# A float32 attention and gated MoE kernel: q and k loaded with their depth in rows, and four low parts of the output weights moved in VectorE's queue

## What is computed

```python
scores = q @ k.transpose(0, 1, 3, 2) / sqrt(D)           # 32 heads, 576 x 576
x      = log1p(abs(i - j)) / log1p(max(i, 1))
bias   = maximum(x[..., None] @ w1 + b1, 0) @ w2         # one bias matrix per head, same for all batches
attn   = softmax(scores + bias)
x      = (attn @ v).transpose(0, 2, 1, 3).reshape(2304, 512)
gate   = sigmoid(x @ w_gate)
out    = (gate * (x @ w_val)) @ w_out
```

## Time and profile before

| | |
|---|---|
| time, median of 3 runs | 765.59 us (764.82 to 766.67) |
| time of the profiled execution | 765.62 us |
| its span, first to last instruction | 763.5 us |
| granted TensorE clock, mean | 0.998 |
| PE busy | 737.0 us, 97% |
| PEld busy | 604.1 us, 79% |
| DVE busy | 508.6 us, 67% |
| ACT busy | 459.0 us, 60% |
| POOL busy | 354.2 us, 46% |
| chain that ended last | PE 84%, DVE 9%, issue 3%, ACT 3%, DMA 1% |

### The profile page before, as it was taken

The page is one execution under the profiler, slowest core; times in us unless marked ns, Lnnn a source line. Parts: engine busy times, 40 slices in busy tenths (PEclk is TensorE's granted clock), DMA queues, the critical chain, the costliest instruction groups (busy, mean ns, idle before and its releaser), DMA issues.

```text
span 763.5 us, 14723 instructions
## 1 busy us (share of the span) xinstructions
PE 737.0 (97%) x5104; PEld 604.1 (79%) x5104; DVE 508.6 (67%) x1082; ACT 459.0 (60%) x939; POOL 354.2 (46%) x483
## 2 busy tenths in 40 slices
PE   7788999999999999999989999999999999999998
PEld 4336777777777767679878998999899889989996
DVE  6996777777777777756950787687068677714851
ACT  6996676776767767657632674375166437615720
POOL 0003454454457787884627562655055265603500
PEclk9999999999999999999999999999999999999999
DMA  6898133232262332113330124222011412200102
GB/s 165 195 217 174 48 80 78 66 77 71 63 200 70 81 77 50 33 44 127 111 110 1 56 83 140 82 60 80 1 57 56 165 59 81 76 8 29 55 4 80
DMA packets 92953, 63.16 MB, mean 83 GB/s; under 512 B 60496, under 2 KB 86224, under 8 KB 92880
## 3 DMA queue, kind: packets, MB, share of 16 engines
q1 hardware_dynamic: 92448, 62.13, 29.7%
q10 hardware_dynamic: 432, 0.09, 0.1%
HBM read 42.15 MB, written 9.44 MB: 68 GB/s over the span
## 4 chain that ended last, share of the span: by engine, by line
PE 84%; DVE 9%; issue 3%; ACT 3%; DMA 1%; POOL 0%; ACTq 0%; DVEq 0%; POOLq 0%
PE f_ps L1421 20%; PE z_ps L1350 18%; PE v_ps L1312 10%; PE y_ps L1350 9%; PE so_ps L1248 7%; DVE feats L942 6%; PE x_ps L1350 4%; PE ty_ps L1261 4%; PE tx_ps L1273 3%; PE so_ps L1243 2%; ACT probs L769 1%; PE tx_ps L1290 1%; PE v_ps L1192 1%; PE ty_ps L1202 1%; PE tx_ps L1278 1%
## 5 line engine op out<-in xcount | busy, mean ns | idle before, releaser
L1350 PE MATMUL z_ps<-xc,wc 128*128 128x384 f32 x864 | 165.3, 336 | 0.2
L588 POOL TENSOR_SCALAR probs<-probs,recip 128x512 f32<-128x512 f32 x128 | 89.2, 697 | 152.3 <-DVE recip L996 152.3
L1350 PEld LDWEIGHTS z_ps<-xc,wc 128*128 128x128 f32 x864 | 150.6, 188 | 3.8 <-ACT keep L796 1.9
L769 ACT ACTIVATE probs<-neg_scores,neg_max 128x576 f32<-128x576 f32 x144 | 111.1, 771 | 61.5 <-DVE neg_max L976 61.5
L976 DVE CUSTOM_DVE_ANT_0 neg_scores<-so_ps,bias 128x576 f32<-128x576 f32 x128 | 91.9, 755 | 3.7 <-PE so_ps L1231 3.2
L614 POOL TENSOR_TENSOR wc<-t_raw,wc 128x512 fp32r<-128x512 f32 x37 | 49.1, 1326 | 88.5 <-ACT wc L788 88.5
L1421 PE MATMUL f_ps<-wo_h,h_h 128*128 128x512 f32 x216 | 85.2, 394 | 2.8 <-issue 2.8
L1350 PE MATMUL y_ps<-xc,wc 128*128 128x384 f32 x432 | 86.7, 335 | 1.0 <-DVE sig L1052 0.5
L1421 PE MATMUL f_ps<-wo_l,h_h 128*128 128x512 f32 x216 | 84.9, 393 | 0.0
L1421 PE MATMUL f_ps<-wo_h,h_l 128*128 128x512 f32 x216 | 84.8, 393 | 0.0
L796 ACT ACTIVATE keep<-z_ps 128x384 f32<-128x384 f32 x108 | 52.9, 490 | 52.4 <-PE z_ps L1350 51.3
(11 more groups left out here) (124 smaller groups left out, 1491.2 us busy)
## 6 DMA issues: line engine op xcount, KB each, us to landing
w_stage<-in_w_gate SPq DMA_DIRECT2D x18, 512.0 KB, 3.6
w_stage<-in_w_val SPq DMA_DIRECT2D x18, 512.0 KB, 3.5
bias<-bias_rows SPq DMA_DIRECT2D x12, 576.0 KB, 6.5
out<-out_sb SPq DMA_DIRECT2D x18, 256.0 KB, 2.0
q_raw<-in_q SPq DMA_DIRECT2D x32, 128.0 KB, 2.8
k_raw<-in_k SPq DMA_DIRECT2D x32, 128.0 KB, 2.6
v_main<-in_v SPq DMA_DIRECT2D x32, 128.0 KB, 2.3
x_whole<-attn_transposed SPq DMA_DIRECT2D x9, 384.0 KB, 4.9
```

The source lines that it names most:

```text
L588: nc.gpsimd.tensor_scalar(row[:, 0:NT * P], row[:, 0:NT * P], by, 1.0, ALU.mult, ALU.mult).then_inc(normed, 1)
L769: nc.scalar.activation(probs[s % RING][:, place, :], neg_scores[:, place, :], ACT.Exp, bias=neg_max[:, stat(s, place)], scale=-1.0, accum_ ...
L1350: last = nc.tensor.matmul(quad_ps[bank][n % 2][:, 0:CH], wc[:, n % 2, wl, W_PARTS.index(wp), t, :], xc[:, X_PARTS.index(x), xl, t, :], sta ...
```

## The change

q and k are laid out anew in DRAM: one array `qk` with, for each of the 16 pairs, 128 rows (the depth of the first head, then of the second) of 1216 columns: 576 of k, 128 of q's last rows (64 for each head, zeros in the other head's columns), 512 of q's other rows. One DMA a pair (`load_qk`, 608 KB, rows of 4864 bytes) brings it into `qk_whole`, which lies at the place of `qk_l`. Nothing is turned on TensorE: the three `turn_` functions and all waits on them, and on the PSUM tiles that they shared, are gone. ScalarE takes the high parts in two pieces from SBUF (`high_qk`, columns 0 to 703 and 704 to 1215), VectorE the low parts in the same two pieces (`low_qk`), in place. For the next pair they stand at steps m=2 and m=3 in both queues, for the first pair at units 7 and 11 (ScalarE), 9 and 13 (VectorE). SyncE issues the load of the next pair at m=0, after a wait for all scores of the pair before. In VectorE's queue of the MoE stage `low_wo` moves from the end of the quad's weight parts to behind `sum_block(n - 1, "12")`. A pad keeps the later tiles at their addresses.

```diff
+            def load_qk(pair):
+                sp.dma_start(qk_whole[pair % 2][:, :], qk[pair, :, :]).then_inc(qk_in[pair % 2], 16)
...
-                if m == 1 and pair + 2 < PAIRS:
-                    sp.wait_ge(tails_turned, pair + 2)
-                    load_qk_tails(pair + 2)
-                if m == 2 and pair + 2 < PAIRS:
-                    sp.wait_ge(k_turned, pair + 2)
-                    load_k(pair + 2)
-                if m == 0 and 1 <= pair < PAIRS - 2:
-                    sp.wait_ge(q_turned, pair + 2)
-                    load_q(pair + 2)
+                if m == 0 and 1 <= pair < PAIRS - 1:
+                    sp.wait_ge(scored, s)
+                    load_qk(pair + 1)
...
+            def high_qk(pair, part):
+                act.wait_ge(qk_in[pair % 2], 16 * (pair // 2 + 1))
                 if pair >= 2:
                     act.wait_ge(scored, SPP * (pair - 1))
+                cols = QK_PARTS[part]
+                nc.scalar.activation(qk_h[pair % 2][:, cols], qk_whole[pair % 2][:, cols], ACT.Copy).then_inc(qk_high, 1)
...
                 if m == 4 and pair >= 1:
                     copy_values(pair - 1)
-                if s == 2:
-                    high_q(1)
-                if m == 4 and pair + 2 < PAIRS:
-                    high_q(pair + 2)
-                if m == 1 and pair + 1 < PAIRS:
-                    high_k(pair + 1)
+                if m in QK_STEPS and pair + 1 < PAIRS:
+                    high_qk(pair + 1, QK_STEPS.index(m))
                 if m != R:
                     for u, place in units[:1]:
                         exponentials(s, u, place)
                 if 0 <= s - LAG < STEPS:
                     move_a(s - LAG)
-                if m == 0 and pair + 1 < PAIRS:
-                    high_tails(pair + 1)
...
+            def low_qk(pair, part):
+                dve.wait_ge(qk_high, 2 * pair + part + 1)
+                cols = QK_PARTS[part]
+                nc.vector.tensor_tensor(qk_l[pair % 2][:, cols], qk_whole[pair % 2][:, cols],
+                                        plain(qk_h[pair % 2][:, cols]), ALU.subtract).then_inc(qk_low, 1)
...
-                if m == 1 and pair + 1 < PAIRS:
-                    low_k(pair + 1)
                 if 0 <= s - LAG < STEPS and (s - LAG) % SPP != R:
                     move_b(s - LAG)
-                if s == 2:
-                    low_q(1)
-                if m == 4 and pair + 2 < PAIRS:
-                    low_q(pair + 2)
+                if m in QK_STEPS and pair + 1 < PAIRS:
+                    low_qk(pair + 1, QK_STEPS.index(m))
                 if m == 1 and pair >= 1:
                     copy_values(pair - 1)
-                if m == 0 and pair + 1 < PAIRS:
-                    low_tails(pair + 1)
...
                 if inside:
                     sum_block(n - 1, "12")
+                for f in WO_LOW.get(n, ()):
+                    low_wo(f)
                 if values:
                     hidden(n - 1, "12")
...
                 if n < QUADS - 1:
                     low_w(n + 1, "B22")
-                for f in WO_LOW.get(n, ()):
-                    low_wo(f)
...
                 if m == 0:
-                    pe.wait_ge(k_low, pair + 1)
-                    pe.wait_ge(tails_low, pair + 1)
-                    pe.wait_ge(q_low, pair + 1)
+                    pe.wait_ge(qk_low, 2 * (pair + 1))
```

More of the change, by code:

```diff
@@ L149, in program @@
         tails_zero = sem("tails_zero")
-        q_in = sem("q_in")
-        k_in = sem("k_in")
-        qk_tails_in = sem("qk_tails_in")
         v_in = [sem(f"v_in{i}") for i in range(2)]
[L154 to L162, removed]
+        qk_in = [sem(f"qk_in{i}") for i in range(2)]
+        qk_high = sem("qk_high")
+        qk_low = sem("qk_low")
         scored_b = sem("scored_b")
@@ L232, in program @@
         neg_scores = sb("neg_scores", [P, 2, S])
-        qk_h = [sb(f"qk_h{i}", [P, Q_MAIN + NT * P], F32R) for i in range(2)]
-        qk_l = [sb(f"qk_l{i}", [P, Q_MAIN + NT * P], F32R) for i in range(2)]
+        qk_h = [sb(f"qk_h{i}", [P, QK_COLS], F32R) for i in range(2)]
+        with ExitStack() as whole_only:
+            qk_whole = [sb(f"qk_whole{i}", [P, QK_COLS], F32, whole_only) for i in range(2)]
+        qk_l = [sb(f"qk_l{i}", [P, QK_COLS], F32R) for i in range(2)]
         v_main = [sb(f"v_main{i}", [P, NT, 2, D]) for i in range(2)]
@@ L490, in store_x @@
                              (x_half0, x_half1)[g][:, :]).then_inc(x_stored[g], 16)
[L492 to L495, removed]
+            load_qk(0)
             sp.dma_start(tail_win[:, :], log_dist_tail).then_inc(tail_win_in, 16)
@@ L498, in _ @@
                 if d == PREP_UNIT // 2 + 2:
[L499 to L504, removed]
+                    load_qk(1)
                 store_bias(d)
@@ L1004, in _ @@
             for u in range(UNITS):
-                if u == PREP_UNIT + 3:
-                    low_q(0)
-                if u == TAILS_UNIT + 3:
-                    low_tails(0)
-                if u == KEYS_UNIT + 3:
-                    low_k(0)
+                if u - 2 in QK_UNITS:
+                    low_qk(0, QK_UNITS.index(u - 2))
                 max_feats(u)
@@ L1257, in transpose_b @@
                     pe.wait_ge(moved_b, pair * NT + m)
-                if m == 0 and pair + 1 < PAIRS:
-                    pe.wait_ge(k_low, pair + 2)
                 for t in range(NT):
@@ L1286, in transpose_r @@
                 pe.wait_ge(moved_a, s)
-                if pair + 2 < PAIRS:
-                    pe.wait_ge(tails_low, pair + 3)
                 for t in range(NT):
@@ L1302, in values @@
                         pe.wait_ge(v_in[i], 16 * V_DMAS * (pair // 2 + 1))
[L1303 to L1305 removed]
+                        if pair >= 1:
                             pe.wait_ge(x_ready[1], pair)
@@ L1371, in _ @@
                     scores(s)
-                if m == 1 and pair + 1 < PAIRS:
-                    turn_k(pair + 1)
                 if s < 2:
@@ L1379, in _ @@
                     values(pair - 1, *VALUE_SLOTS[m])
-                tails_of = pair + 1 if m == 0 and pair + 1 < PAIRS else None
                 if 0 <= c < STEPS and c % SPP == R:
@@ L1384, in _ @@
                     transpose_b(c)
-                    if s == 2:
-                        turn_q(1)
-                    if m == 4 and pair + 2 < PAIRS:
-                        turn_q(pair + 2)
-                    transpose_a(c, tails_of)
-                elif tails_of is not None:
-                    turn_tails(tails_of)
+                    transpose_a(c)
                 if m in (0, 2, 3) and pair >= 1:
@@ L1473 @@
     w2_sets = w2_sets.reshape(P, GRP * H)
-    arrays = {"q": q, "k": k, "v": v, "hidden_wb": hidden_wb, "w2_sets": w2_sets, "w_gate": moe_w_gate,
+    qk = np.zeros((PAIRS, 2, D, QK_COLS), dtype=q.dtype)
+    q_rows = q.reshape(PAIRS, 2, S, D).transpose(0, 1, 3, 2)
+    qk[:, :, :, 0:S] = k.reshape(PAIRS, 2, S, D).transpose(0, 1, 3, 2)
+    qk[:, :, :, Q_MAIN:] = q_rows[:, :, :, 0:NT * P]
+    for j in range(2):
+        qk[:, j, :, Q_TAIL + j * REM:Q_TAIL + (j + 1) * REM] = q_rows[:, j, :, NT * P:S]
+    qk = qk.reshape(PAIRS, P, QK_COLS)
+    arrays = {"qk": qk, "v": v, "hidden_wb": hidden_wb, "w2_sets": w2_sets, "w_gate": moe_w_gate,
               "w_val": moe_w_val, "w_out": moe_w_out, "log_dist": log_dist, "inv_log_pos": inv_log_pos,
```

117 lines of the change are left out of this document (11 added, 106 removed).

## The result

The changed kernel takes 757.4 us (median of 6 runs, 755.89 to 757.92), the kernel before, on the same chip, 766.12 us (6 runs, 764.82 to 768.87): a ratio of 0.9883, 95% interval 0.9867 to 0.9900. The forecast was 757.1. The profiled execution of the changed kernel took 755.89 us with a span of 754.1, against 763.5 of span before; its granted clock is 0.995 in the mean.

The account below looks back on a forecast made before the run. TensorE was taken to bound attention and MoE, with a latency loop of VectorE and ScalarE close below. From 765.62 us: -8.7 + 3.6 + 1.2 + 0 - 4.65 = -8.5, giving 757.1 us; range 750.0 to 762.3.

Parts of the forecast that it names:

- The cycle of a pair: Attention, pairs 0 to 8: longest cycle of waits sums to 16.04 us a pair against 17.01, nine pairs -8.7 us.
- Pair 0 and the high and low parts there: Attention: pair 0 gains 0.97 like the others; ScalarE's and VectorE's larger pieces fit, else up to 0.9 us a pair.
- Pair 9: Attention: the load for pair 10 lands behind a 2.5 MB burst, ScalarE waits, pair takes 20.6 us, +3.6.
- The first rival: Load for pair 10 in time or ScalarE's wait absorbed: pair 9 like 10, -3.5, total 753.6 us; chance 0.17.
- The port in pairs 10 to 14: Attention: VectorE's low parts and GpSimd exclude each other in SBUF; pairs take 17.1 to 17.2 us, +1.2 in all.
- The sign that was named: Late attention pairs: VectorE's low parts would take 1.5 us and more from step 47 on.
- The start: Bias stage: taken as 0, bounds -0.6 to +1 us, the latter for the larger first load beside small ones.
- The low parts of the output weights: MoE stage: moving low_wo removes the 2.83 us wait before first outputs and 1.82 of half clock, -4.65 us.
- That the port costs nothing: Low parts slip between GpSimd's pieces, pairs 9 to 14 gain 0.97 each, total 750.3 us; chance 0.12.
- That the MoE wait only moves: MoE stage: wait shifts to weights behind low_wo and to hidden values, total 761.8 us; chance 0.10.
- That the loop of VectorE and ScalarE holds the pairs: Attention: each pair held at 5 x 3.37, nine pairs bring 1.4 instead of 8.7, total 764.4 us; chance 0.08.
- That the load is late in every pair: Attention: slower; landing of 9.5 us would give 771, each further us costing one in 14 pairs; chance 0.05.

## Why the prediction was right, and where it was not

The main mechanism was right, and so was that of pair 9; three sizes were off. The closeness of the sum is luck, as the errors of the terms cancel.

**The cycle of a pair: right.** 16.04 was worked out, 15.98 came, and the chain has the pieces that were summed. The runs with transposes on it and off it show that it binds, by 0.09 us over a second one (an estimate: 16.33 less the 0.44 of the transposes). That second one had not been seen; it had no effect, as the longest was the right one.

**Pair 0 and the high and low parts there: right.** Both fit under the cover that was named; `low_qk` takes 0.88 (rows above), and `add_eps` in pairs 1 to 8 waits for ScalarE as before.

**Pair 9: right, and by its mechanism.** 20.6 was worked out, from a landing behind the burst; it took 20.72, in other runs 20.46 to 22.12, and 16.28 when the load went ahead of the burst. In the run of 22.12 the clock is at 0.50 for 6 us behind the wait, in the changed kernel for 2 to 3. The first rival, that the load is in time, is out. By the Trainium skill, DMA: Bandwidth & Descriptors, section "Queues, rings and completion order", descriptors of a queue are taken in ring order; the run with the load ahead agrees: landing after 4.2 us in place of 8.8, and the loads then behind it later by 1.1 to 1.4. Of the 4.4 us that the pair got shorter, a part is the earlier issue.

**The port in pairs 10 to 14: right in kind, mis-sized.** The step that failed is "the other and then `add_eps` come behind both: 2.4 + 1.0 + 0.88 = 4.3 us instead of 3.37". It let GpSimd's piece go first. In the rows `low_qk` starts 0.08 us ahead of it at m=2 (255.85 and 255.93), so it is not lengthened at all, and only `add_eps` meets the end of the piece: 0.34 to 0.53 us more at m=2, not 0.9, and 0.14 to 0.43 at m=3, not 0.7. The sign that was named, low parts of 1.5 us and more, didn't come. The pairs take 16.28 to 17.26 us, 16.71 in the mean, where 17.1 to 17.2 was forecast: 2.0 to 2.5 us over five pairs. The rest of the miss is the base: the forecast set 17.1 to 17.2 against 17.01, but pairs 12 to 14 took 17.77, 17.25 and 17.31 before, 1.3 us more, with collisions of their own. The forecast of +1.2 for these pairs became -2.8, and -2.2 with pair 15, within the bounds that were given. Pair 15 stood in no term of the sum: it got 0.62 us longer in this profile, and 1.9 where it takes 18.25. The sentence in the forecast that the operation waits "for GpSimd's to end" holds for `add_eps`, but who starts first had to be read from the queues, 1.1 us ahead of `add_eps`; the prediction took the worse case. The Trainium skill, SBUF — State Buffer, section "SBUF: two separate sides", says that whichever starts first has the port for its whole instruction. The rows of pair 11 and of the run with additional work agree: `low_qk` takes its 0.88 us, and GpSimd's operation 1.67 for 1.02.

**The start: wrong.** 0 was taken, with bounds of -0.6 and +1, and it is +2.69 in the profile, 2.5 in the mean of all profiles. The text named "the larger first load beside the small ones" and gave it at most 1 us without a row. What the rows of before offered was there: `log_win` landed in 4.3 us and the small loads beside it in 4.5 and 4.7, and no price was formed for 608 KB more in front of them. The run with the load later shows it whole.

**The low parts of the output weights: right in kind, mis-sized.** Forecast -4.65, measured -3.87 from the end of pair 15, and a stage shorter by 3.5 to 3.7 by undoing it and doing it alone. The step "up to 1.4 later if it meets GpSimd ... I take no wait at all" failed: the two tiles took 3.34 us instead of 1.28, 2.06 more, and 0.65 of wait stayed. P1 at n=4 waits 0.53 us; up to 0.8 was counted in the bounds for it, nothing in the sum. The half clock behind the idle time did go: 4.58 to 2.99.

**The rivals.** That the port costs nothing is out by the run with additional GpSimd work. That the MoE wait only moves is out by the stage's 3.5 to 3.7 us, though 0.53 of new wait stands at n=4. That the loop of VectorE and ScalarE holds the pairs is out in pairs 1 to 8. That the load is late in every pair is out: the median landing is 4.9 us.

## What to carry to other kernels

Before one stage's work is taken off the bounding engine, follow the next cycle piece by piece, as here: it gave 16.04 for 15.98, where TensorE's own time would have promised 0.4 us more in each. The new layout saved work on TensorE and put one large load where seven small ones had been, which cost time in the queues: ask of each large load what is ahead of it, behind it and beside it, above all at the very start and beside a burst. Here the two places cost 2.5 and 4.4 us beside a gain of 8.7, and two edits of SyncE's queue brought them back, less 1.7 us that pairs 10 and 15 gave up again in the profiles. When two engines exclude each other, read from the queues which one starts first, and look at the short operation behind both.

## What was not expected of the hardware

A waiting VectorE operation was not let in between GpSimd operations that followed each other without a gap: `add_eps` of 0.17 us took 2.44, through two whole operations (1.03 and 1.30 us) that started after it. With no piece at step 74, pair 15 took 16.77 us in place of 18.24.

A 1 KB load on ScalarE's queue landed after 5.8 us instead of 4.1, and one of 16 KB after 6.6 instead of 3.7, when SyncE's queue had 608 KB more to move in the meantime; that one edit is the difference between the two runs.

Open: why the first microseconds differ from run to run (slow first matmuls in nine of thirteen profiles, in six of them with the clock shown at 0.50), and with it up to 1.5 us of the start; why pair 13 took 17.35 and 16.66 in the same attention code; and what decides between 17.0 and 18.25 us in pair 15 of the same code.
